# Masked attention on one core: scores issued one unit ahead, the row normalisation moved to the head of VectorE's step, a padded tail of the values, and a scan cut into pieces

## The reference

```python
scores = scale * np.matmul(q, k.transpose(0, 1, 3, 2))
thresh = np.max(scores, axis=-1, keepdims=True) - tau
scores = np.where(scores >= thresh, scores, -1000000000.0)
scores = scores - np.max(scores, axis=-1, keepdims=True)
attn = np.exp(scores)
attn = attn / (np.sum(attn, axis=-1, keepdims=True) + 1e-09)
return np.matmul(attn, v)
```

## Time and profile before

| | us |
|---|---|
| median of 3 runs (1223.11 to 1231.73) | 1229.59 |
| the profiled execution, its own time | 1223.09 |
| its span, first to last instruction | 1221.4 |
| PE busy | 972.1 (80%) |
| PEld (weight loads) busy | 793.6 (65%) |
| DVE busy | 768.8 (63%) |
| ACT busy | 546.8 (45%) |
| POOL busy | 397.0 (33%) |

### The profile page before, as it was taken

One profiled execution on the slowest core, in us unless ns is written; L12 is line 12 of the kernel. 1 busy time (PEld: TensorE's weight loads), 2 busy tenths in 40 slices (PEclk: granted clock), 3 DMA queues, 4 the chain that ended last, 5 costly groups with the idle time before them and its releaser, 6 DMA issues. The chain is left out here.

```text
span 1221.4 us, 17758 instructions
## 1 busy us (share of the span) xinstructions
PE 972.1 (80%) x5988; PEld 793.6 (65%) x5988; DVE 768.8 (63%) x1336; ACT 546.8 (45%) x842; POOL 397.0 (33%) x319
## 2 busy tenths in 40 slices
PE   4788868968886861787887787787776599999997
PEld 3577757757675651565666666666655497978785
DVE  6576666676656531878888887878885444444442
ACT  5565545545544511554555564555553331313130
POOL 2444325324331203433434552543452030303010
PEclk9899989998998965888888897888888799999999
DMA  4332212311320331300441432440000402010101
GB/s 115 79 80 60 61 45 80 103 51 48 92 50 12 95 132 62 129 29 20 173 156 35 167 126 68 163 167 20 26 14 0 170 1 79 1 67 12 39 1 39
DMA packets 48562, 87.53 MB, mean 72 GB/s; under 512 B 6700, under 2 KB 17324, under 8 KB 48240
## 3 DMA queue, kind: packets, MB, share of 16 engines
q1 hardware_dynamic: 41760, 74.83, 19.5%
q0 software_dynamic: 5584, 9.74, 2.4%
q10 hardware_dynamic: 1152, 2.10, 0.6%
...
## 5 line engine op out<-in xcount | busy, mean ns | idle before, releaser
L873 DVE TENSOR_TENSOR w_low<-w,w_high 128x1024 fp32r<-128x1024 f32 x150 | 273.9, 1837 | 94.3 <-ACT w_high L972 93.4
L972 ACT CAST w_high<-w 128x1024 fp32r x200 | 209.6, 1049 | 206.5 <-PE ps_y L1129 159.7
L627 DVE TENSOR_REDUCE max_tau<-ps_s 128x1 f32<-128x576 f32 x144 | 108.1, 750 | 128.7 <-PE ps_s L473 128.6
L446 ACT COPY probs_t<-ps_ring 128x512 f32<-128x512 f32 x192 | 104.7, 563 | 143.6 <-PE ps_ring L518 134.9
L1129 PE MATMUL ps_y<-w_high,hidden_t_low 128*128 128x512 f32 x200 | 82.0, 499 | 91.4 <-DVE hidden_t_low L1038 91.2
L873 POOL TENSOR_TENSOR w_low<-w,w_high 128x1024 fp32r<-128x1024 f32 x50 | 126.0, 2547 | 2.8 <-ACT w_high L972 1.8
L550 PE MATMUL ps_ring<-probs_t,v_pair 128*64 128x144 f32 (+1 forms) x1280 | 104.2, 301 | 27.9 <-DVE w L666 14.6
L472 PE MATMUL ps_s<-w_in_low,w_in_high 128*128 128x288 f32 x336 | 109.8, 344 | 16.9 <-DVE w_in_high L607 12.3
L397 ACT ACTIVATE w<-ps_s,max_tau 128x576 f32<-128x576 f32 x144 | 108.2, 752 | 29.5 <-DVE max_tau L627 29.2
L1129 PEld LDWEIGHTS ps_y<-w_high,hidden_t_low 128*128 128x128 f32 x200 | 46.5, 246 | 111.5 <-DVE hidden_t_low L1038 102.2
L550 PEld LDWEIGHTS ps_ring<-probs_t,v_pair 128*64 128x64 f32 (+1 forms) x1280 | 74.5, 139 | 55.7 <-DVE w L666 20.3
...
...
## 6 DMA issues: line engine op xcount, KB each, us to landing
w<-in_w SPq DMA_DIRECT2D x16, 2048.0 KB, 12.3
...
```

The costliest lines, as they stand in the source:

```text
L446: nc.scalar.copy(out, src).then_inc(evacuated, 1)
L627: nc.vector.tensor_reduce(max_tau[:, n % 4, 0:1], scores(n), AX_XY, ALU.max, negate=True).then_inc(maxed, 1)
L873: return engine.tensor_tensor(w_parts[1][j][:], raw, w_parts[0][j][:].bitcast(F32), ALU.subtract)
L972: nc.scalar.copy(w_parts[0][j][:], raw).then_inc(chunk_high, 1)
```

## The change

It has five parts.

1. `score(0)` is issued before the loop, and TensorE's step n issues `score(n + 1)` ahead of the ring's items of step n. Its wait is the same: unit n-2 must be masked before the scores of n+1.
2. In VectorE's step the normalisation of the last piece stands ahead of the row maximum.
3. The last 64 rows of values are loaded into their own half only, the other half holds zeros from the start (four memsets of 64x64), and the last chunk of a piece uses all 128 partitions, with 128 by 64 tiles as the others.
4. The scan is cut. VectorE keeps the two scan instructions and the product: `choose` in step 23, `rank_tokens` in step 26. The first three elementwise instructions become two, on GpSimd: `keep_codes`, between `spread` and `split_q`, and `hot_codes`, behind `split_q`.
5. With `add` and `min` in place of `mult` and `add` the first scan reads the codes themselves, so that one mask is no longer needed.

The diff, without declarations:

```diff
--- before.py
+++ after.py
@@ -67,7 +67,7 @@
 TAIL_AT = 2 * FULL * S
 SPAN = 2 * S + 2 * TAIL
 MAIN_AT, TAILS_AT, SUMS_AT, REST_AT, PV_AT = 3, W + 2, W + 4, W + 5, W + 6
-LOGITS_AT, ARGMAX_AT, SPREAD_AT, SCAN_AT, CHOSEN_AT, PROB_AT = 12, 16, 19, 21, 28, 30
+LOGITS_AT, ARGMAX_AT, SPREAD_AT, CHOOSE_AT, RANK_AT, CHOSEN_AT, PROB_AT = 12, 16, 19, 23, 26, 28, 30
 ROWS_AT = (21, 23, 30, 32, 33)
 
 
@@ -261,7 +262,8 @@
             sp.dma_start(dst[:, 0:FULL, :], v_dram[batch, 0:FULL * P, cols].rearrange("(t p) d -> p t d", p=P)).then_inc(v_loaded[pair % 2], 16)
             for half in range(2):
 
-                sp.dma_start(dst[TAIL * half:TAIL * half + TAIL, FULL, :], v_dram[batch, FULL * P:S, cols]).then_inc(v_loaded[pair % 2], 16)
+                own = slice(DH * half, DH * half + DH)
+                sp.dma_start(dst[own, FULL, own], v_dram[batch, FULL * P:S, 2 * DH * j + DH * half:2 * DH * j + DH * half + DH]).then_inc(v_loaded[pair % 2], 16)
 
         def store_rows(b):
 
@@ -355,6 +357,20 @@
                                   inv_sum[:, 0:2 * FULL].unsqueeze(2).to_broadcast([P, 2 * FULL, DH]))
             nc.gpsimd.tensor_copy(inv_cols[:, FULL, :], inv_sum[:, W - 1:W].to_broadcast([P, P])).then_inc(spread_out, 1)
 
+        def keep_codes(b):
+
+            pool.wait_ge(evacuated, out_of_ring("spread", 1, b))
+            nc.gpsimd.tensor_scalar(keep[:], code_r[:], float(E), float(E), ALU.is_lt, ALU.mult).then_inc(kept, 1)
+
+        def hot_codes(b):
+
+            if b == 0:
+                pool.wait_ge(consts, POOL_CONSTS + DVE_CONSTS)
+            else:
+                pool.wait_ge(turned, filled("place", 0, b - 1))
+            pool.wait_ge(chosen, b + 1)
+            nc.gpsimd.tensor_scalar(onehot[:], chosen_r[:], expert_id[:, 0:1], None, ALU.is_equal).then_inc(hot, 1)
+
         def scatter_ids(b):
 
             pool.wait_ge(evacuated, out_of_ring("place", 0, b))
@@ -378,11 +394,17 @@
                 split_k(pair + 1)
             if pair > 0:
                 spread(pair - 1)
+            if pair % PAIRS == 2 and pair > PAIRS:
+                keep_codes(pair // PAIRS - 1)
             if pair + 1 < ALL_PAIRS:
                 split_q(pair + 1)
+            if pair % PAIRS == 2 and pair > PAIRS:
+                hot_codes(pair // PAIRS - 1)
             if pair % PAIRS == PAIRS - 1 and pair > PAIRS:
                 scatter_ids(pair // PAIRS - 1)
         spread(ALL_PAIRS - 1)
+        keep_codes(B - 1)
+        hot_codes(B - 1)
         scatter_ids(B - 1)
 
     @block.scalar
@@ -545,9 +567,8 @@
                 pt, v, cols = probs_t[of % 2], v_pair[of % 2], slice(PIECE * i, PIECE * i + PIECE)
                 for c in range(QT):
                     for h in range(2):
-                        part = slice(0, P) if c < FULL else slice(DH * h, DH * h + DH)
                         chunk = FULL * h + c if c < FULL else W - 1
-                        last = nc.tensor.matmul(bank[DH * h:DH * h + DH, 0:PIECE], v[part, c, DH * h:DH * h + DH], pt[part, chunk, cols],
+                        last = nc.tensor.matmul(bank[DH * h:DH * h + DH, 0:PIECE], v[:, c, DH * h:DH * h + DH], pt[:, chunk, cols],
                                                 start=(c == 0), stop=(c == QT - 1))
             elif kind == "logits":
                 if i == 0:
@@ -579,9 +600,11 @@
             last.then_inc(turned, 1)
 
         pe.wait_ge(const_loaded, 48)
+        pe.wait_ge(v_padded, 4)
+        score(0)
         for n in range(len(STEPS)):
-            if n < UNITS:
-                score(n)
+            if n + 1 < UNITS:
+                score(n + 1)
             for k, item in enumerate(STEPS[n]):
                 fill(FIRST_OF_STEP[n] + k, item)
 
@@ -597,6 +620,10 @@
     def _(dve):
         nc.vector.memset(q_split[0][:, S:S + TAIL].bitcast(F32), 0.0).then_inc(set_up, 1)
         nc.vector.memset(q_split[1][:, S:S + TAIL].bitcast(F32), 0.0).then_inc(set_up, 1)
+        for i in range(2):
+
+            for h in range(2):
+                nc.vector.memset(v_pair[i][DH * (1 - h):DH * (1 - h) + DH, FULL, DH * h:DH * h + DH], 0.0).then_inc(v_padded, 1)
         dve.wait_ge(k_loaded, 32)
         nc.vector.tensor_copy(k_high[0][:], k_in[:]).then_inc(k_cast, 1)
         dve.wait_ge(k_cast, 1)
@@ -694,25 +721,18 @@
             nc.vector.scalar_tensor_tensor(out=code8[:], in0=code_b[:].unsqueeze(2).to_broadcast([P, QT, E]), scalar=100.0,
                                            in1=fresh[:].unsqueeze(2).to_broadcast([P, QT, E]), op0=ALU.add, op1=ALU.add).then_inc(coded, 1)
 
-        def scan(b):
-
-            dve.wait_ge(evacuated, out_of_ring("spread", 1, b))
+        def choose(b):
+
+            dve.wait_ge(kept, b + 1)
+            nc.vector.tensor_tensor_scan(chosen_r[:], keep[:], code_r[:], 0.0, ALU.add, ALU.min).then_inc(chosen, 1)
+
+        def rank_tokens(b):
+
+            dve.wait_ge(hot, b + 1)
+            nc.vector.tensor_tensor_scan(rank[b % 2][:], ones_r[:], onehot[:], rank[1 - b % 2][:, S - 1:S], ALU.mult, ALU.add).then_inc(counted, 1)
             if b > 0:
                 dve.wait_ge(turned, filled("place", 0, b - 1))
-            n0 = b * SCAN_STEPS
-            count = [0]
-
-            def step(ins):
-                count[0] += 1
-                ins.then_inc(scan_step, 1)
-                dve.wait_ge(scan_step, n0 + count[0])
-
-            step(nc.vector.scalar_tensor_tensor(out=keep[:], in0=code_r[:], scalar=float(E), in1=ones_r[:], op0=ALU.is_equal, op1=ALU.mult))
-            step(nc.vector.scalar_tensor_tensor(out=renew[:], in0=code_r[:], scalar=float(E), in1=code_r[:], op0=ALU.is_lt, op1=ALU.mult))
-            step(nc.vector.tensor_tensor_scan(chosen_r[:], keep[:], renew[:], 0.0, ALU.mult, ALU.add))
-            step(nc.vector.scalar_tensor_tensor(out=onehot[:], in0=chosen_r[:], scalar=expert_id[:, 0:1], in1=ones_r[:],
-                                                op0=ALU.is_equal, op1=ALU.mult))
-            step(nc.vector.tensor_tensor_scan(rank[b % 2][:], ones_r[:], onehot[:], rank[1 - b % 2][:, S - 1:S], ALU.mult, ALU.add))
+            dve.wait_ge(counted, b + 1)
             nc.vector.scalar_tensor_tensor(out=placed[:], in0=rank[b % 2][:], scalar=region_at[:, 0:1], in1=onehot[:],
                                            op0=ALU.add, op1=ALU.mult).then_inc(ranked, 1)
 
@@ -737,12 +757,12 @@
 
         for n in range(len(STEPS)):
             pair, w = unit_of(n)
-            if n < UNITS:
-                row_max(n)
             if n > 0:
                 for k, item in enumerate(STEPS[n - 1]):
                     if item[0] == "pv":
                         pv_normalise(FIRST_OF_STEP[n - 1] + k, item)
+            if n < UNITS:
+                row_max(n)
             if 0 < n <= UNITS:
                 mask(n - 1)
             if n < UNITS:
@@ -753,8 +773,10 @@
             b, at = divmod(n, PAIRS * W)
             if b > 0 and at == ARGMAX_AT:
                 argmax(b - 1)
-            if b > 0 and at == SCAN_AT:
-                scan(b - 1)
+            if b > 0 and at == CHOOSE_AT:
+                choose(b - 1)
+            if b > 0 and at == RANK_AT:
+                rank_tokens(b - 1)
             if b > 0 and at == PROB_AT:
                 if b == B:
```

9 lines of the change are left out of this document (5 added, 4 removed).

## The result

The changed kernel takes 1181.44 us (median of 4 runs, 1179.45 to 1187.7) against 1228.34 us (4 runs, 1223.11 to 1231.73) of the kernel before beside it: a ratio of 0.963, 95% interval 0.958 to 0.9681. Profile against profile it is 1181.42 for 1223.09, 41.7 us less. Of these 40.8 lie in the attention stage, which now ends (with the last indirect DMA of the token numbers) at 421.77 us for 462.57.

What follows compares the result with a forecast made beforehand. No engine was full; waits between engines bound attention's steps. Gains of 4.5, 9, 27, 6.7, 0.5 and -0.8 sum to 46.9 us, taking 1223.1 to 1176; two added for a median gave 1178, range 1148 to 1205.

Steps and rivals of the forecast that it cites:

- plain pairs: Attention pairs 2, 3, 4, 8, 12, without logits or scan: 0.9 us gained each, to 20.4, five giving 4.5.
- pairs 7, 11 and 15: Attention pairs behind the scan, and the last: 2.6 us gained in 7 and 11, 1.5 in 15, together 6.7.
- The pv step: Attention steps with a pv piece: TensorE's own work alone closes the chain, 2.45 us in place of 3.38.
- The loop: Mask, scores, transposes, copy, exponential, mask: 3.42 us, spanning two units instead of three, costing about 2.8 a plain pair.
- rival that it holds nobody: Attention's mask-to-mask loop delays no engine: 1.9 us more gained on 15 pairs, 28 in all, 1149; chance 15%.
- A pass with a second copy: One turn from mask to mask where ScalarE copies two items: 1.95 us a unit instead of 1.71.
- Pairs with logits: Attention pairs 5, 9 and 13, with a batch's logits: 3.0 us gained each, 9 in all, bounds 0.9 and 5.
- The scan: Pairs 6, 10 and 14: cutting the scan gains 9.0 us a pair, 27 in all, bounds 7 and 11 a pair.
- GpSimd's masks: The scan's two tensor_scalar masks on GpSimd: 1.9 us each, ends 0.7 and 4.
- The end: Last batch, uncovered: scan stretch 8.2 us for 6.0, 2.1 slower; four pv pieces win 1.3; net -0.8.
- The rival of 18%: TensorE's clock falls in the new waits of attention steps without pieces: 26 us more, 1204; chance 18%.
- the one on the other side: Slower than before: clock stays at 1.2 GHz into pv steps, 4.9 us each for 2.45, near 1300; chance 4%.

Runs made afterwards that it cites:

- kernel without part 1: Changed kernel with TensorE issuing the scores of unit n in step n again, rest kept: 1159.93 us, 0.9508 of before; run again 1162.26 us, 0.9477.
- split one score later: Changed kernel with GpSimd's split of k waiting for one more unit's scores: 1172.52 us, 0.9588 of the kernel before.

## Why the prediction was right

The time came at 1181.44 for 1178. The sum did less well than that looks: 46.9 us were forecast from profile to profile, 41.7 came. (The medians, 1228.34 and 1181.44, do lie 46.9 apart, but only because the profiled execution of before was the fastest of its runs while that of after is its median; two errors of 5 us met.) By the table of pairs the sum put the plain pairs 2.1 too high, those with logits 4.6, the scan 1.5, pairs 7, 11 and 15 2.0, and the end 3.5 too low. That the total lies 3.4 us off is in part luck, since most of those 3.5 are the clock's (below).

**The pv step**: mechanism right, 2.54 for 2.45. Twenty loads and the switch back took 1.38, as the sum 1.14 + 0.17 has it but for 0.07. Right too that the normalisation is no longer waited for, and that the padding costs nothing per load: 0.16 is saved by it. What the prediction did not say is that this gain needs no scores ahead. It gave it to both parts together; the runs show that each takes the wait away by itself, part 2 at no price and part 1 for the loop.

**The loop**: there, at the links that were named. The rival that it holds nobody had 15%; it is what the kernel without part 1 does, with 18.66 us a plain pair where the prediction put 18.5 for no loop. The loop took 2.1 from a plain pair, and the gain left was 0.49 for the forecast 0.9. The prediction's own split of that 0.9, four steps that win 0.93 and 2.8 given back, does not fit its 18.5 for no loop. The first piece of a pair never waited for a normalisation (its load at 109.09 in the kernel before follows ScalarE after 0.17), so three steps win 0.93. That is 2.8 won and 1.9 given back, and the runs have 2.6 and 2.1. A pass with a second copy was put at 3.9 (twice 1.95) and takes 3.90 (102.84 to 106.74, mask to mask). Followed by the starts of the scores, the nine steps were forecast as 2.45 1.95 1.8 2.2 1.5 2.4 2.5 3.2 2.4 and came as 2.54 1.88 1.74 2.44 1.47 2.43 2.54 3.22 2.54. The 0.4 that is missing are 0.3 of switches and loads in the four `pv` steps and 0.24 in the step behind ScalarE's scaling and two copies, less 0.13 elsewhere.

**Pairs with logits**, 4.4 for 9: this step failed. It took these pairs as plain pairs with TensorE's own work added, and did not ask what else the earlier score releases. `scored` is also GpSimd's signal to start on the next k, and that ran into the argmax. One score more in that wait gives 10.2, so the sum was about right for a kernel in which nothing else hangs on that count. A part of the 10.2 is the clock: before, it fell in each of these pairs (mean 0.94), with the split one score later only in pair 9. Pairs 7, 11 and 15, 4.7 for 6.7, were not looked into further.

**The scan**, 25.5 for 27: right, with pairs at 25.4, 23.9 and 22.9 for the 23.5 or so forecast, and the wait of 6.8 is gone. Pair 6 still opens at the low clock from pair 5 (a first step of 4.14 for 2.56 in pairs 10 and 14). `choose` took 1.33 or 1.34 in all three batches and ran beside no GpSimd instruction. What the prediction named as a sign of being wrong, `rank_tokens` waiting for GpSimd, did come in part, in the first two batches. The first:

```profile
163.72 1.40 DVE L732 TENSOR_TENSOR_SCAN rank<-ones_r,rank,onehot 8x576 f32<-8x576 f32 x1
163.92 2.40 POOL L337 TENSOR_TENSOR w_in_high<-w,w_in_low 128x576 fp32r<-128x576 f32 x1
165.15 1.78 DVE L736 SCALAR_TENSOR_TENSOR placed<-rank,region_at,onehot 8x576 f32<-8x576 f32 x1
```

The product took 1.78 there and 1.71 in the second batch, for 0.81 in the third, and each time ended 0.6 behind GpSimd's instruction. The step is 4.83 and 4.91 long for 3.92, so it cost about 1 us each time.

**GpSimd's masks** took 2155 ns and 1734 ns on average (groups of the profile):

```profile
L363 POOL TENSOR_SCALAR keep<-code_r 8x576 f32<-8x576 f32 x4 | 8.6, 2155 | 18.3 <-ACT code_r L468 18.0
L372 POOL TENSOR_SCALAR onehot<-keep,expert_id 8x576 f32<-8x576 f32 x4 | 6.9, 1734 | 9.5 <-DVE keep L727 9.5
```

The 1.9 taken from the earlier trace rows lies between them. (Its 1.68 is a mean over two shapes, with 1.56 as the middle value.) The line rate that the Trainium skill (GPSIMD Engine Reference, 3.1 and 4.1) gives, 0.5 by the prediction's estimate, does not fit: both took over three times as long. The last batch's stretch was 7.8 for 8.2.

**The end** gained 2.7 where -0.8 was forecast. The two `pv` steps ahead of the last pieces gave 1.1, which the sum had left out; the four pieces in a row 1.0 (5.12 for 6.16) for the 1.3 forecast; the masks cost 1.8 for 2.1. The remaining 2.3 are the clock: 1.7 in the logits (4.52 for 6.21) and 0.6 in the transposes behind them, since TensorE ran at the lower level from 435.5 to 446 before and from about 397 to 401 after. That is luck rather than the change: in two executions of the same kernel without part 1 the same forty matmuls took 6.19 and 4.27.

**The clock** did not fall in the new waits: the five plain pairs run at 1.00 with waits of up to 1.21 in them. It rose in the pairs with the scan, from 0.89 or 0.90 to 0.94, 1.00 and 1.00. Before, each of them had a stretch of about 7 us at the lower level behind the wait of 6.79, and that is gone. The rival of 18% and the one on the other side had the price of a mechanism that did not start at waits of this length. Longer waits did not decide it alone either. In pair 9 the piece waited as long for the argmax as in pair 5, and the scores behind it ran at full clock; in the kernel before the clock fell in pair 5 with no wait over 0.63 ahead of it, right behind the first matmuls of the routing. The rows, first of after, then of before:

```profile
237.23 1.45 PE L571 MATMUL ps_ring<-probs_t,v_pair 128*64 128x144 f32 x20 [1.85 <-DVE w L693]
238.63 0.40 PE L494 MATMUL ps_s<-w_in_low,w_in_high 128*128 128x288 f32 x1
```

```profile
125.96 3.01 PE L558 MATMUL ps_ring<-w_route,w 128*128 128x9 f32 x24
128.82 0.59 PE L472 MATMUL ps_s<-w_in_low,w_in_high 128*128 128x288 f32 x1
```

Why it falls in one pair and not in the next, these runs do not show.
